# 132 matmuls on constant tiles ahead of the first real matmul of an attention and two-MLP kernel

## The chip, the cores and the metric

The kernel runs on one core of one Trainium2 chip. The metric is the device time of one execution in microseconds (us), the median of the runs made of it.

## The reference

Queries `q` of 12,288 tokens with 128 channels attend to 768 keys. The keys are the mean over 4 x 4 windows of `kv`, multiplied by `w_sr`, and serve as values too. The result goes through two MLPs of 128 -> 2048 -> 128, one with a ReLU whose negative side has a slope `alpha` per feature, one with a sigmoid approximation of GELU.

```python
kv_pool = kv.reshape(B, H // r, r, W // r, r, C).mean(axis=(2, 4))   # r = 4
k = v = kv_pool.reshape(B, -1, C) @ w_sr
a = softmax(q @ k.T / sqrt(C))
x = a @ v
h = x @ w_in;  y = (maximum(h, 0) + alpha * minimum(h, 0)) @ w_out
h = y @ w_in2; out = (h * sigmoid(1.702 * h)) @ w_out2
```

All tensors are float32.

## The kernel before, in words

Everything is held transposed, with the 128 channels on the partitions. The 12,288 tokens are worked off in 24 tiles of 512. Each of the five engines has one hand-written stream of instructions, and semaphores tie the streams together; nothing is reordered by a scheduler. So what stands first in an engine's stream holds up everything behind it on that engine.

A real product is made of three matmuls on float32r parts (`passes`, lines 639 to 641): high weights by high data, high by low, low by high. Each is 128 x 512 and brings a weight load of its own (engine PEld in the profile).

The program has a head and a loop. The head works in this order:

- SP loads `kvT` in 12 chunks of 512 KB into a ring of four buffers (`kv_raw`, line 234). From the fifth chunk on, each load waits until the chunk four before it has been reduced (`pooled_made`). Behind the last chunk come `w_in1`, `w_out1` and the second tile of queries (lines 241, 242, 245).
- DVE reduces each chunk to 64 keys (line 590). Behind chunk 3, 5, 7, 9 it makes the low parts of keys and values of a pair of chunks (`keys_values_lo`, lines 485 and 487), which waits for ACT's high parts. Behind chunk 4 it makes the high part of the first queries (line 480), from which POOL makes `q_lo` (line 277).
- PE multiplies each pair of chunks by `w_sr` (`keys_values`, lines 649 and 650, 128 x 128), and then makes the scores of the first query tile for the pair before (`scores`). ACT copies the products out and makes the high parts (lines 335, 336, 339).
- Then follow the maximum over the keys, the exponentials, attention of the first tile, the turned weights `w_in1` (line 772) and their product with `w_out1` (`mix`, line 701), and the first three `up` products, with which the steady part begins.

The loop then runs `tile` over the 24 tiles. In it the MLPs of tile t and the attention of tile t + 1 are interleaved on PE.

POOL begins its own stream with the identity matrix `ident` (memset at line 263, then 265), used by transposes much later. PE begins with `pe.wait_ge(small_in, 2 * DMA)` and `keys_values(0)`. The PSUM banks `ps_t` and `ps_y` (one bank each) are first used at lines 670 and 701.

Of the kernel before, what the change touches and what calls it, by code (L numbers as in the profile page):

```python
# [6 lines left out]
F32R = mybir.dt.float32r  # L7
# [4 lines left out]
P = 128  # L12
POOL = 4
WINDOW = POOL * POOL
TOK = 512
# [9 lines left out]
def attention_mlp_kernel(  # L25
# [53 lines left out]
    with ExitStack() as ctx:  # L79
        def sb(name, shape, dt=F32):  # L80
            return ctx.enter_context(nc.sbuf_tensor(name, shape, dt))

        def psum(name, shape):
            return ctx.enter_context(nc.psum_tensor(name, shape, F32))

        def sem(name):
            return ctx.enter_context(nc.semaphore(name))
# [4 lines left out]
        ps_t = psum("ps_t", [P, 512])  # L92
        ps_y = psum("ps_y", [P, 512])


        ident = sb("ident", [P, P])
        alpha_sb = sb("alpha_sb", [P, CH])
        one_less = sb("one_less", [P, CH])
# [53 lines left out]
        y_free = sem("y_free")  # L152
        mix_split = sem("mix_split")
        ident_made = sem("ident_made")
        warm_made = sem("warm_made")
        up1_hi_made = sem("up1_hi_made")
        pooled_made = sem("pooled_made")
# [46 lines left out]
        def f32(ap):  # L204
            return ap.bitcast(F32)
# [19 lines left out]
        @block.sync  # L225
        def _(sp):

            sp.sem_inc(out_free, DMA)
            for c in range(KV_CHUNKS):
                if c >= KV_RING:  # L230

                    sp.wait_ge(pooled_made, c - KV_RING + 1)
                src = kvT[:, c * KV_KEYS * WINDOW:(c + 1) * KV_KEYS * WINDOW]
                sp.dma_start(kv_raw[:, c % KV_RING].rearrange("p k w -> p (k w)"),
                             src).then_inc(kv_in[c % KV_RING], DMA)
                if c == 0:
                    sp.dma_start(wsr_sb[:], w_sr).then_inc(small_in, DMA)
                    sp.dma_start(alpha_sb[:], alpha).then_inc(small_in, DMA)
                if c == 1:
                    sp.dma_start(q_raw[:], qT[:, 0:TOK]).then_inc(q_in, DMA)  # L240
            sp.dma_start(w_raw[0][:], w_in1).then_inc(w_in[0], DMA)
            sp.dma_start(w_raw[1][:], w_out1).then_inc(w_in[1], DMA)

            sp.wait_ge(q_split, 1)
            sp.dma_start(q_raw[:], qT[:, TOK:2 * TOK]).then_inc(q_in, DMA)

            sp.wait_ge(w_hi, 1)
            sp.wait_ge(up0_lo_made, 1)
            sp.wait_ge(w_turned, RING)
            sp.dma_start(w_raw[0][:], w_in2).then_inc(w_in[2], DMA)  # L250

            sp.wait_ge(down0_lo_made, 1)
            sp.dma_start(w_raw[1][:], w_out2).then_inc(w_in[3], DMA)

            with sp.Fori(0, TILES - 2) as t:

                sp.wait_ge(q_split, t + 2)
                sp.dma_start(q_raw[:], qT[:, bass.ds(t * TOK + 2 * TOK, TOK)]).then_inc(q_in, DMA)


        @block.gpsimd
        def _(pool):
            nc.gpsimd.memset(ident[:], 0.0).then_inc(ident_made, 1)
            pool.wait_ge(ident_made, 1)
            nc.gpsimd.affine_select(out=ident[:], in_=ident[:], compare_op=ALU.not_equal, fill=1.0, base=0,
                                    pattern=[[-1, P]], channel_multiplier=1).then_inc(ident_made, 1)

            def scale_rows(src, factors, dst):

                src, dst = (w[:].rearrange("p (j c) -> p j c", j=CH) for w in (src, dst))  # L270
                by = factors[:].rearrange("p (j o) -> p j o", o=1).broadcast_to([P, CH, C])
                return nc.gpsimd.tensor_tensor(dst, src, by, ALU.mult)

            def queries_lo(u):

                pool.wait_ge(q_hi_made, u + 1)
                nc.gpsimd.tensor_tensor(q_lo[:], q_raw[:], f32(q_hi[:]), ALU.subtract).then_inc(q_split, 1)  # L277

            def subtract_max(u):

                pool.wait_ge(max_out, u + 1)
                for c in range(KC):
                    nc.gpsimd.tensor_tensor(s_sb[:, c, :], s_sb[:, c, :], max_sb[:], ALU.subtract).then_inc(  # L283
                        diff_done, 1)

            def sum_exponentials(u):
                for c in range(1, KC):

                    pool.wait_ge(exp_done, u * KC + (c + 1))
                    if c > 1:  # L290

                        pool.wait_ge(exp_sum_done, u * (KC - 1) + (c - 1))
                    nc.gpsimd.tensor_tensor(exp_sum[:], s_sb[:, 0, :] if c == 1 else exp_sum[:], s_sb[:, c, :],  # L293
                                            ALU.add).then_inc(exp_sum_done, 1)

            nc.gpsimd.memset(warm[:], 0.0).then_inc(warm_made, 1)
            queries_lo(0)

            pool.wait_ge(w_in[1], DMA)
            scale_rows(w_raw[1], alpha_sb, scaled).then_inc(w_scaled, 1)  # L300
            pool.wait_ge(alpha_made, 1)
            pool.wait_ge(w_scaled, 1)
            scale_rows(w_raw[1], one_less, w_raw[1]).then_inc(w_scaled, 1)

            sum_exponentials(0)
            queries_lo(1)

            pool.wait_ge(w_hi, 2)
            nc.gpsimd.tensor_tensor(down_lo[0][:], w_raw[1][:], f32(down_hi[0][:]), ALU.subtract).then_inc(
                down0_lo_made, 1)  # L310

            pool.wait_ge(up1_hi_made, 1)
            nc.gpsimd.tensor_tensor(up_lo[1][:], w_raw[0][:], f32(up_hi[1][:]), ALU.subtract).then_inc(mlp2_parts, 1)

            pool.wait_ge(w_in[3], DMA)
            nc.gpsimd.tensor_copy(down_hi[1][:], w_raw[1][:]).then_inc(mlp2_parts, 1)
            pool.wait_ge(mlp2_parts, 2)
            nc.gpsimd.tensor_tensor(down_lo[1][:], w_raw[1][:], f32(down_hi[1][:]), ALU.subtract).then_inc(
                mlp2_parts, 1)
            with pool.Fori(1, TILES - 1) as u:  # L320
                subtract_max(u)
                sum_exponentials(u)
                queries_lo(u + 1)
            subtract_max(TILES - 1)
            sum_exponentials(TILES - 1)
# [310 lines left out]
        def _(pe):  # L636
# [129 lines left out]
            def turn_w_in1(g):  # L766
# [5 lines left out]
                    step = nc.tensor.transpose(w_turn_bank(g)[:, cols(j % 4)], w_raw[0][:, cols(j)], ident[:])  # L772
                step.then_inc(w_turned, 1)

            pe.wait_ge(small_in, 2 * DMA)
            for c in range(KC):
                keys_values(c)
# [65 lines left out]
```

## Time and profile before

| what | us |
|---|---|
| median of the runs (2) | 1409.12 |
| lowest and highest | 1408.65, 1409.59 |
| span of the profiled execution, first to last instruction | 1407.1 |
| PE busy in it | 1365.1 (97%) |
| DVE busy | 1088.8 (77%) |
| ACT busy | 823.9 (59%) |
| POOL busy | 444.9 (32%) |

The profiled execution has 1407.1 us as its span; the median lies 2.0 us above it. A matmul's duration in the profile includes the part in which the next one already runs, so the time that a matmul costs in a stream is the distance between two starts. L with a number is the line of the kernel. PEclk is the granted clock of TensorE, 1.00 being 2.4 GHz and 0.50 being 1.2 GHz.

### The profile page before, as it was taken

What the parts mean: (1) busy time and instruction counts of PE and PEld (TensorE: products, weight loads), DVE (VectorE), ACT (ScalarE), POOL (GpSimd) and SP (SyncE); (2) the same over time, 40 slices, a digit from 0 to 9 for tenths busy, and PEclk for the clock granted to TensorE, in tenths of its full rate; (3) what the DMA queues carried; (4) which work ended last, traced back from release to release, by engine and by line L of the source; (5) the groups of instructions that cost most, each with busy time, mean ns of one, the idle gap of its engine ahead of it and who ended that gap; (6) DMA issues with size and microseconds to landing.
All of it is one profiled execution on the core that took longest, in us unless ns stands there. A gap on an engine that the chain in (4) does not pass through costs nothing.

```text
span 1407.1 us, 19487 instructions
## 1 busy us (share of the span) xinstructions
PE 1365.1 (97%) x6000; PEld 1094.6 (78%) x6000; DVE 1088.8 (77%) x1689; ACT 823.9 (59%) x1417; POOL 444.9 (32%) x295
## 2 busy tenths in 40 slices
PE   4599999999999999999999999999999999999998
PEld 3477887887887878878878788788787787887776
DVE  6868878778678787787786887877968877778775
ACT  2465665656656656656566566565665665655644
POOL 2740522413405314234054142241440522413400
PEclk8699999999999999999999999999999999999999
DMA  7100000000000000000000000000000000000000
GB/s 255 68 1 16 0 15 15 0 15 7 7 15 7 7 15 0 15 7 7 15 7 7 15 0 15 15 0 15 7 7 15 0 15 15 0 15 0 8 8 8
DMA packets 9514, 23.26 MB, mean 17 GB/s; under 512 B 1184, under 2 KB 1312, under 8 KB 8992
## 3 DMA queue, kind: packets, MB, share of 16 engines
q1 hardware_dynamic: 6048, 16.85, 3.6%
q10 hardware_dynamic: 3456, 6.29, 1.2%
q8 instruction: 4, 0.07, 0.0%
q14 instruction: 6, 0.05, 0.0%
HBM read 16.85 MB, written 6.29 MB: 16 GB/s over the span
## 4 chain that ended last, share of the span: by engine, by line
PE 90%; DVE 6%; ACT 1%; DMA 1%; issue 0%; SPq 0%; DVEq 0%; ACTq 0%
PE ps_y L639 14%; PE ps_y L641 13%; PE ps_y L640 13%; PE ps_h L641 12%; PE ps_h L639 12%; PE ps_h L640 12%; PE ps_s L639 4%; PE ps_s L640 4%; PE ps_s L641 4%; DVE g_lo L545 3%; PE ps_t L670 2%; PE ps_t L682 2%; DMA kv_raw<-kvT 1%; ACT g_full L372 1%; DVE g_hi L543 1%; DVE wide L502 0%
## 5 line engine op out<-in xcount | busy, mean ns | idle before, releaser
L283 POOL TENSOR_TENSOR s_sb<-s_sb,max_sb 128x512 f32<-128x512 f32 x138 | 205.3, 1523 | 577.6 <-ACT max_sb L349 577.6
L537 DVE SCALAR_TENSOR_TENSOR g_lo<-ps_h,g_hi 128x512 fp32r<-128x512 f32 x384 | 264.0, 688 | 153.1 <-ACT g_hi L367 150.5
L372 ACT ACTIVATE g_full<-ps_h 128x512 f32<-128x512 f32 x384 | 229.8, 598 | 252.6 <-PE ps_h L641 247.6
L545 DVE TENSOR_TENSOR g_lo<-g_full,g_hi 128x512 fp32r<-128x512 f32 x384 | 309.6, 806 | 13.1
L639 PE MATMUL ps_y<-g_hi,down_hi 128*128 128x512 f32 x768 | 313.4, 408 | 1.6 <-DVE g_lo L545 0.5
L641 PE MATMUL ps_y<-g_hi,down_lo 128*128 128x512 f32 x768 | 303.4, 395 | 0.0
L640 PE MATMUL ps_y<-g_lo,down_hi 128*128 128x512 f32 x768 | 302.4, 394 | 0.0
L367 ACT ACTIVATE g_hi<-ps_h 128x512 fp32r<-128x512 f32 x384 | 229.1, 597 | 94.2 <-PE ps_h L641 81.7
L543 DVE CAST g_hi<-g_full 128x512 fp32r<-128x512 f32 x384 | 161.9, 422 | 28.1 <-ACT g_full L372 28.0
L639 PEld LDWEIGHTS ps_y<-g_hi,down_hi 128*128 128x128 f32 x768 | 144.7, 188 | 47.7 <-DVE g_lo L545 18.6
L515 DVE TENSOR_TENSOR a_lo<-s_sb,a_hi 128x512 fp32r<-128x512 f32 x144 | 171.3, 1190 | 1.2 <-ACT a_hi L362 1.2
L641 PEld LDWEIGHTS ps_y<-g_hi,down_lo 128*128 128x128 f32 x768 | 144.3, 188 | 33.9
L640 PEld LDWEIGHTS ps_y<-g_lo,down_hi 128*128 128x128 f32 x768 | 144.7, 188 | 29.1
L639 PE MATMUL ps_h<-x_hi,up_hi 128*128 128x512 f32 x384 | 153.9, 401 | 1.6 <-DVE x_lo L551 1.6
L639 PE MATMUL ps_h<-y_hi,up_hi 128*128 128x512 f32 x384 | 151.1, 393 | 1.5 <-DVE y_lo L569 1.5
L641 PE MATMUL ps_h<-x_hi,up_lo 128*128 128x512 f32 x384 | 151.7, 395 | 0.0
L641 PE MATMUL ps_h<-y_hi,up_lo 128*128 128x512 f32 x384 | 151.6, 395 | 0.0
L640 PE MATMUL ps_h<-y_lo,up_hi 128*128 128x512 f32 x384 | 151.6, 395 | 0.0
L640 PE MATMUL ps_h<-x_lo,up_hi 128*128 128x512 f32 x384 | 151.0, 393 | 0.0
L293 POOL TENSOR_TENSOR exp_sum<-exp_sum,s_sb 128x512 f32<-128x512 f32 x96 | 142.0, 1479 | 10.7 <-ACT s_sb L354 2.6
L344 ACT COPY s_sb<-ps_s 128x512 f32<-128x512 f32 x144 | 84.5, 587 | 86.7 <-PE ps_s L641 74.7
L277 POOL TENSOR_TENSOR q_lo<-q_raw,q_hi 128x512 fp32r<-128x512 f32 x24 | 33.5, 1394 | 281.6 <-DVE q_hi L480 281.6
(90 smaller groups left out, 1774.9 us busy)
## 6 DMA issues: line engine op xcount, KB each, us to landing
kv_raw<-kvT SPq DMA_DIRECT2D x12, 512.0 KB, 5.4
q_raw<-qT SPq DMA_DIRECT2D x24, 256.0 KB, 2.6
outT<-out_sb ACTq DMA_DIRECT2D x24, 256.0 KB, 2.0
w_raw<-w_in SPq DMA_DIRECT2D x2, 1024.0 KB, 6.2
w_raw<-w_out SPq DMA_DIRECT2D x2, 1024.0 KB, 7.3
wsr_sb<-w_sr SPq DMA_DIRECT2D x1, 64.0 KB, 3.2
alpha_sb<-alpha SPq DMA_DIRECT2D x1, 8.0 KB, 3.5
```

The source lines that it names most:

```text
L283: nc.gpsimd.tensor_tensor(s_sb[:, c, :], s_sb[:, c, :], max_sb[:], ALU.subtract).then_inc(diff_done, 1)
L293: nc.gpsimd.tensor_tensor(exp_sum[:], s_sb[:, 0, :] if c == 1 else exp_sum[:], s_sb[:, c, :], ALU.add).then_inc(exp_sum_done, 1)
L344: nc.scalar.copy(s_sb[:, c, :], score_bank(c)).then_inc(scores_out, 1)
L367: nc.scalar.activation(g_hi[:, f % RING, :], ps_h[:, f % RING, :], ACT.Relu).then_inc(act_done, 1)
L372: nc.scalar.activation(g_full[:, f % RING, :], ps_h[:, f % RING, :], ACT.Gelu_apprx_sigmoid).then_inc(act_done, 1)
L515: nc.vector.tensor_tensor(a_lo[:, c % A_RING, :], s_sb[:, c, :], f32(a_hi[:, c % A_RING, :]), ALU.subtract).then_inc(a_split, 1)
L537: nc.vector.scalar_tensor_tensor(g_lo[:, f % RING, :], ps_h[:, f % RING, :], 0.0, f32(g_hi[:, f % RING, :]), ALU.max, ALU.subtract).then_i ...
L543: nc.vector.tensor_copy(g_hi[:, f % RING, :], g_full[:, f % RING, :]).then_inc(gelu_hi_made, 1)
L545: nc.vector.tensor_tensor(g_lo[:, f % RING, :], g_full[:, f % RING, :], f32(g_hi[:, f % RING, :]), ALU.subtract).then_inc(g_split, 1)
L639: nc.tensor.matmul(out, w_hi_ap, m_hi_ap, start=start, stop=False)
L640: nc.tensor.matmul(out, w_hi_ap, m_lo_ap, start=False, stop=False)
L641: return nc.tensor.matmul(out, w_lo_ap, m_hi_ap, start=False, stop=stop)
```

## The change

Two constant tiles are made by POOL ahead of the identity matrix: `probe_w`, two 128 x 128 weight tiles filled with 1.0, and `probe_m`, two 128 x 512 data tiles filled with 0.5. PE waits for both and then streams 132 matmuls of 128 x 512 on them into `ps_t` and `ps_y`, whose contents nothing reads. The six streams are:

1. 20 matmuls, weights in turn, one data tile, one bank;
2. 20 matmuls, weights and data in turn, one bank;
3. 20 matmuls, weights in turn, banks in turn;
4. 8 triples that accumulate like `passes`, banks in turn;
5. 8 triples with a semaphore signal behind each;
6. 8 triples with the signal and a wait that is already met.

Behind them the program of before goes on unchanged. No other engine's stream is changed.

```diff
+        probe_w = sb("probe_w", [P, 2, P], F32R)
+        probe_m = sb("probe_m", [P, 2, TOK], F32R)
         ident = sb("ident", [P, P])
...
+        probe_made = sem("probe_made")
+        probe_streamed = sem("probe_streamed")
...
         @block.gpsimd
         def _(pool):
+            nc.gpsimd.memset(f32(probe_w[:]), 1.0).then_inc(probe_made, 1)
+            nc.gpsimd.memset(f32(probe_m[:]), 0.5).then_inc(probe_made, 1)
             nc.gpsimd.memset(ident[:], 0.0).then_inc(ident_made, 1)
...
+            def stream(count, w, m, out):
+                for i in range(count):
+                    nc.tensor.matmul(out(i)[:], probe_w[:, w(i), :], probe_m[:, m(i), :], start=True, stop=True)
+
+            def triples(count, signal, wait):
+                for i in range(count):
+                    j = 0
+                    out = (ps_t, ps_y)[i % 2]
+                    if wait:
+                        pe.wait_ge(probe_made, 2)
+                    nc.tensor.matmul(out[:], probe_w[:, j, :], probe_m[:, j, :], start=True, stop=False)
+                    nc.tensor.matmul(out[:], probe_w[:, j, :], probe_m[:, j + 1, :], start=False, stop=False)
+                    step = nc.tensor.matmul(out[:], probe_w[:, j + 1, :], probe_m[:, j, :], start=False, stop=True)
+                    if signal:
+                        step.then_inc(probe_streamed, 1)
+
+            pe.wait_ge(probe_made, 2)
+            stream(20, lambda i: i % 2, lambda i: 0, lambda i: ps_t)
+            stream(20, lambda i: i % 2, lambda i: i % 2, lambda i: ps_t)
+            stream(20, lambda i: i % 2, lambda i: 0, lambda i: (ps_t, ps_y)[i % 2])
+            triples(8, False, False)
+            triples(8, True, False)
+            triples(8, True, True)
+
             pe.wait_ge(small_in, 2 * DMA)
             for c in range(KC):
                 keys_values(c)
```

The stream of PE at its very start, in the kernel before, with the semaphores that it waits for:

```order
L635 UNCONDITIONAL_BRANCH [waits barrier_Pool_Activation_PE_DVE_SP_release]
L649 MATMUL ps_h<-pooled,wsr_sb 128x128 [waits pooled_made,small_in]
L650 MATMUL ps_h<-wsr_sb,pooled 128x128
L649 MATMUL ps_h<-pooled,wsr_sb 128x128 [waits pooled_made]
L650 MATMUL ps_h<-wsr_sb,pooled 128x128
L639 MATMUL ps_s<-q_hi,k_hi 128x512 [waits kv_lo,q_split]
```

The same place in the changed kernel, whose lines 655, 656 and 645 are lines 649, 650 and 639 of before:

```order
L641 UNCONDITIONAL_BRANCH [waits barrier_Pool_Activation_PE_DVE_SP_release]
L784 MATMUL ps_t<-probe_m,probe_w 128x512 [waits probe_made]
L784 MATMUL ps_t<-probe_m,probe_w 128x512 x40
L784 MATMUL ps_y<-probe_m,probe_w 128x512
...
L792 MATMUL ps_y<-probe_m,probe_w 128x512 [waits probe_made]
L793 MATMUL ps_y<-probe_m,probe_w 128x512
L794 MATMUL ps_y<-probe_m,probe_w 128x512
L655 MATMUL ps_h<-pooled,wsr_sb 128x128 [waits pooled_made,small_in]
L656 MATMUL ps_h<-wsr_sb,pooled 128x128
L655 MATMUL ps_h<-pooled,wsr_sb 128x128 [waits pooled_made]
L656 MATMUL ps_h<-wsr_sb,pooled 128x128
L645 MATMUL ps_s<-q_hi,k_hi 128x512 [waits kv_lo,q_split]
```

The first `keys_values` product stands behind all 132 matmuls, in an unchanged order from there on.

The stream of DVE at its start, the same in both kernels, here in the kernel before; `kv_in` is a chunk's landing and `kv_hi` counts ACT's copies of PE's products:

```order
L472 UNCONDITIONAL_BRANCH [waits barrier_Pool_Activation_PE_DVE_SP_release]
L590 TENSOR_REDUCE pooled<-kv_raw 128x64 [waits kv_in0]
L600 TENSOR_SCALAR one_less<-alpha_sb 128x16 [waits small_in]
L590 TENSOR_REDUCE pooled<-kv_raw 128x64 [waits kv_in1]
L590 TENSOR_REDUCE pooled<-kv_raw 128x64 [waits kv_in2]
L590 TENSOR_REDUCE pooled<-kv_raw 128x64 [waits kv_in3]
L485 TENSOR_TENSOR k_lo<-k_full,k_hi 128x128 [waits kv_hi]
L487 SCALAR_TENSOR_TENSOR v_lo<-ps_h,v_hi 128x128
L590 TENSOR_REDUCE pooled<-kv_raw 128x64 [waits kv_in0]
L480 CAST q_hi<-q_raw 128x512 [waits q_in]
L590 TENSOR_REDUCE pooled<-kv_raw 128x64 [waits kv_in1]
```

Nothing moved here; the wait for `kv_hi` behind the fourth reduction is where DVE meets PE's first product.

## Rows read from the trace of the kernel before

**Rows 1.** The page: span, and busy time by engine.
```profile
span 1407.1 us, 19487 instructions
PE 1365.1 (97%) x6000; PEld 1094.6 (78%) x6000; DVE 1088.8 (77%) x1689; ACT 823.9 (59%) x1417; POOL 444.9 (32%) x295
```

**Rows 2.** Busy time by stretch: PE, PEld, DVE, ACT, POOL (count), PEclk, DMA, GB/s.
```profile
60.00:75.00 15.00, 9.18 (x43) 8.37 (x44) 11.47 (x7) 3.16 (x6) 10.27 (x3) 0.77 0.25 88
75.00:100.00 25.00, 25.00 (x113) 20.35 (x112) 18.19 (x26) 16.69 (x31) 10.67 (x8) 1.00 0.00 1
```

**Rows 3.** Chain that ended last, 0 to 60 us: start, duration, what.
```profile
3.62 7.25 DMA kv_raw<-kvT
...
24.71 1.22 DVE pooled L590
```

**Rows 4.** Timeline of 0 to 20 us: start, duration, engine, line, operation.
```profile
0.74 0.20 POOL L263 MEMSET ident<- 128x128 f32 x1 [0.29 <-POOLq L836]
...
1.43 0.10 POOL L296 MEMSET warm<- 128x1 f32 x1
...
8.64 0.76 PE L649 MATMUL ps_h<-pooled,wsr_sb 128*128 128x128 f32 x2 [8.64 <-DVE pooled L590]
...
9.62 2.49 DVE L590 TENSOR_REDUCE pooled<-kv_raw 128x64 f32<-128x1024 f32 x2 [1.13 <-DMA kv_raw<-kvT]
9.92 1.28 ACT L335 ACT_TABLE_LOAD   x1 [9.92 <-PE ps_h L650]
...
12.23 0.28 DVE L487 SCALAR_TENSOR_TENSOR v_lo<-ps_h,v_hi 128x128 fp32r<-128x128 f32 x1
12.43 1.21 DVE L590 TENSOR_REDUCE pooled<-kv_raw 128x64 f32<-128x1024 f32 x1
...
14.06 1.26 POOL L277 TENSOR_TENSOR q_lo<-q_raw,q_hi 128x512 fp32r<-128x512 f32 x1 [12.54 <-DVE q_hi L480]
15.02 0.45 DVE L485 TENSOR_TENSOR k_lo<-k_full,k_hi 128x128 fp32r<-128x128 f32 x1
15.38 0.29 PEld L639 LDWEIGHTS ps_s<-q_hi,k_hi 128*128 128x128 f32 x1 [2.28 <-POOL q_lo L277]
...
16.82 0.63 PE L649 MATMUL ps_h<-pooled,wsr_sb 128*128 128x128 f32 x2
...
18.25 0.30 ACT L339 CAST k_hi<-k_full 128x128 fp32r<-128x128 f32 x1
...
19.61 0.43 SPq L241 DMA_DIRECT2D w_raw<-w_in  x1
```

**Rows 5.** PE's timeline in the loop, first and last of 37 matmuls.
```profile
599.63 0.39 PE L640 MATMUL ps_y<-g_lo,down_hi 128*128 128x512 f32 x1
...
607.99 0.39 PE L640 MATMUL ps_s<-a_lo,v_hi 128*128 128x512 f32 x1
```

**Rows 6.** PE's timeline in the head at the low clock.
```profile
49.02 0.63 PE L640 MATMUL ps_s<-a_lo,v_hi 128*128 128x512 f32 x1
...
49.45 0.63 PE L641 MATMUL ps_s<-a_hi,v_lo 128*128 128x512 f32 x1
```

**Rows 7.** Timeline of the head: where bursts of PE begin, and line 641 at 21.14.
```profile
21.14 0.46 PE L641 MATMUL ps_s<-q_hi,k_lo 128*128 128x512 f32 x1
...
46.13 0.80 PE L639 MATMUL ps_s<-a_hi,v_hi 128*128 128x512 f32 x1 [1.28 <-DVE a_lo L515]
...
64.20 1.12 PE L682 MATMUL ps_t<-ident,wide 128*128 128x128 f32 x4 [7.28 <-DVE wide L502]
```

**Rows 8.** Busy time by stretch of 1 us (columns as in rows 2), two queries.
```profile
55.00:56.00 1.00, 1.00 (x6) 0.81 (x6) 0.74 (x2) 0.00 (x0) 1.00 (x1) 0.80 0.00 0
...
69.00:70.00 1.00, 0.84 (x7) 0.65 (x6) 1.00 (x1) 0.13 (x1) 1.00 (x1) 0.97 0.00 0
```

**Rows 9.** DMA issues on the page: count, size, median us to landing.
```profile
kv_raw<-kvT SPq DMA_DIRECT2D x12, 512.0 KB, 5.4
```

**Rows 10.** Costliest groups on the page: a weight load of the second MLP product.
```profile
L641 PEld LDWEIGHTS ps_y<-g_hi,down_lo 128*128 128x128 f32 x768 | 144.3, 188 | 33.9
```

## The prediction, made before the changed kernel ran

> **What bounds the kernel now.** I read the page first. The span is 1407.1 us and PE is busy in 97% of it [rows 1]. Next the busy time by stretch: from 75 us on PE is busy without a gap (25.00 of 25.00 us) at granted clock 1.00, while between 60 and 75 us it has work for 9.18 of 15 us [rows 2]. So there are two regimes. In the loop PE is the bound, and whatever arrives late at the loop's door moves the end by as much. In the head PE mostly waits, and delay on it may be swallowed. The change stands in the head, so the question is how much slack the head has ahead of PE's first product. The chain that ended last says what the head hangs on: the landing of the kv chunks from 3.62 us (a piece of 7.25 us first), up to the twelfth reduction, DVE's at 24.71 us, ending at 25.93 [rows 3]. Last I read the timeline of the first 20 us to see which engine feeds which [rows 4].
>
> **The change part by part.** Nothing is removed. Added are two memsets on POOL, 132 matmuls with their weight loads on PE, and a wait of PE for the memsets.
>
> *Memsets.* POOL's memset of 128 columns takes 0.20 us, that of 1 column 0.10, so about 0.10 fixed and 0.8 ns a column [rows 4]. 256 columns give 0.30 and 1024 give 0.91 us. They begin where `ident` began, at 0.74, so PE starts its stream near 0.74 + 0.30 + 0.91 + 0.05 = 2.0 us. POOL's subtraction over 512 columns takes 1.26 us, 2.5 ns a column [rows 4]; at that rate the memsets end at 3.9, the upper bound; the lower is 1.0, were they done as fast as `ident`'s. I take 2.0, since the same operation is the nearest row. `ident` and all else on POOL come about 1.2 us later, hidden: POOL idles from 1.5 to 14.06, waiting for DVE [rows 4].
>
> *A matmul at the high clock.* In the loop 37 starts in a row lie between 599.63 and 607.99: 8.36 / 36 = 0.232 us each [rows 5]. They are the same 128x512 with one weight load each, so I take 0.232. Below, 512 columns at 2.4 GHz are 0.213 us. Above, if each had to end before the next starts, it would be the row's duration of 0.39; the rows speak against that, since starts lie closer than durations.
>
> *A matmul at the low clock.* Starts at 49.02 and 49.45, so 0.43 [rows 6]; 512 columns at 1.2 GHz are 0.427.
>
> *How long the stream runs at the low clock.* A burst that begins at 64.20 after 7.28 us of idleness runs unbroken, and in the stretch 69 to 70 the granted clock is 0.97, which puts the rise at 69.06: 4.9 us [rows 7, 8]. A burst with gaps beginning at 46.13 saw the rise in 55 to 56 (0.80: at 55.4), 9.3 us on. The first rise must come near 21.1, where line 641 shortens from 0.63 to 0.46 us [rows 7], 5.8 us behind the scores' start at 15.38. What stands recorded as 1.00 before that can't be so: spacings there are those of 1.2 GHz. I take 4.9 us, the unbroken burst being nearest to a stream without gaps; bounds 0 and 9.3.
>
> *The six streams together.* 4.9 us hold 11.4 matmuls at 0.427. The other 120.6 at 0.232 take 28.0 us. Together 32.9 us; PE is free at T = 2.0 + 32.9 = 34.9 us. Order of weights, data and banks, the signals and the met waits I cost at nothing: real triples with different operands, banks, signals and waits already run at 0.232.
>
> The Trainium skill, "TensorE: Matmul & The Clock Gate", section "Wait — 56ns, not 53.3ns?", says that back-to-back starts at the full clock lie N / 2.4 GHz plus about 2.5 ns apart, 215.7 ns at N = 512. The loop's 0.232 doesn't agree. By the page's figure the stream would be about 2.0 us shorter; that is the first rival below.
>
> *What the delay of the first product costs.* PE's first product moves from 8.64 to 34.9 [rows 4], 26.3 us. Part comes back, since four chunks are already reduced, and four more landed, when PE arrives. DVE ends its fourth reduction at 9.62 + 2.49 = 12.1 as before, and then stands at `keys_values_lo(0)`, which needs ACT, which needs PE. Behind DVE the eight other reductions wait, behind those SP's loads of chunks 8 to 11, and behind these both weight loads. I replay the head with durations of before [rows 4], counted from T:
>
> - first product at the high clock done at 0.65 (low: 9.92 - 8.64 = 1.28). ACT's table load and copies, then `v_lo` ends at 12.51 - 9.92 = 2.6 later, less 0.2 since DVE isn't late: 3.1.
> - reduction 5, `q_hi`, reduction 6 as before (12.51 to 15.02): 5.6. `q_lo` starts 1.55 after `v_lo`'s end and takes 1.26: scores begin at 6.0.
> - `keys_values_lo(1)` 0.45, reductions 7 and 8: 8.5. `keys_values_lo(2)` needs the third pair's `k_hi`, 18.55 - 15.38 = 3.2 after the scores' start, at the low clock: 9.2.
> - to 9.65; two reductions to 12.1; `keys_values_lo(3)` to 12.55; the last two reductions to 15.0.
>
> Do the loads keep up? The loads of chunks 8 to 11 are issued at 4.3, 5.6, 7.3 and 8.5. At the median of 5.4 us to landing, which they had under full traffic [rows 9], they land at 9.7, 11.0, 12.7 and 13.9, against use at 9.65, 10.9, 12.55 and 13.8: at most 0.2 us late. The load of `w_in1` follows 6.1 us ahead of the last reduction's end; before it was 25.93 - 19.61 = 6.3 [rows 3, 4]. So from there on the head is as it was.
>
> The last reduction ends at 34.9 + 15.0 = 49.9 instead of 25.93: +24.0 us, and 2.3 of the 26.3 us come back. The rest of the head, the loop and the end are the same, all later by 24.0. Phases of the clock in the head may add or take 1.5 us.
>
> **The sum.** 1407.1 + 24.0 = 1431.1 us of span, and with the 2.0 us by which the median stands above this span, 1433.1 us, 1.7% over 1409.1. A change of 2%, about what a measurement of this kernel can tell from no change, is 28.2 us: 1437.3.
>
> **The rivals.**
>
> *The stream runs at 0.213.* The loop's extra 0.019 us would then come from signals, waits or traffic of other engines, which plain constants lack. Against it: nothing in the timeline sits between the 37 starts, and triples are among the probes. 120.6 x 0.019 is 2.3 us less: 1430.8 us. Chance 0.15.
>
> *The starts come closer than 512 columns at 2.4 GHz.* If two matmuls could overlap until the weight load bounds them, its 0.188 us [rows 10], the 120.6 take 22.7 instead of 28.0 us and the time is 1427.8. Against it: the loop's dense rows keep 0.232 with the same weight load. Chance 0.02. The Trainium skill, the same page, section "Back-to-back issue gap", gives 131 ns a matmul at N = 512 as sustained; an estimate by that page would be 1421 us. The loop's 0.232 [rows 5] disagrees with it.
>
> *The clock stays low, on the slower side.* Were the clock not raised in the stream, or taken back within it, each matmul costs 0.427: all 132 take 56.4 us, T is 58.4 and the time 1433.1 + 23.5 = 1456.6. It passes 1437.3 as soon as the low clock lasts 9 us longer than my 4.9, about 14 us in all. For it: the clock fell in the head several times and a rise came after 9.3 us once. Against it: the stream has no gap, and in the loop the clock stays at 1.00. Chance 0.07.
>
> *The head swallows less.* If the shift of 26.3 us comes through whole, 1435.4 us. If late memsets (+1.9 us), a late rise (+2.0) and late chunks come on top, it goes to 1439. Chance 0.15.
>
> *The head swallows all.* It would need the chain of landings to stay the later of the two. But T lies 9 us behind the last reduction of before, and eight reductions and all scores still come behind T. 1409 us. Chance 0.01.
>
> **How the numbers follow.** The forecast with its own spread (1432 to 1435) has 0.60. The range goes from the fast stream with an early rise, 1428.5, to late memsets and a late rise together, 1439. It leaves out the low clock, the closest starts and the swallowed delay, and a small rest of the others. Slower by over 2%: 0.07 for the low clock, 0.05 of the case of the head that swallows less, 0.01 of the rest, 0.13. Faster by over 2%: nothing is taken off the path, 0.01. Within 2%: 0.86.
>
> **What would show it.** Right: PE's first probe near 2 us; starts of 0.43 for some 5 us, then 0.232 in all six streams; the first product of line 655 near 35 us; four reductions by 12 us, then DVE idle until about T + 2.6; the last reduction near 50; the loop's spacing unchanged and every stage later by the same 24 us. Wrong: a stream that differs from the others in spacing, a granted clock of 0.50 past 14 us, a late last chunk, or a loop whose length changes. A shift at the loop's door other than 24 us while T is 35 would refute the replay of the head.

## The result, and the profile after

The changed kernel takes 1431.91 us (median of 2 runs, 1431.54 to 1432.29) against 1409.12: ratio 1.0162, 95% interval 1.0143 to 1.0181. It is 22.8 us slower, where 24.0 were forecast, inside the range of 1428.5 to 1439. The profiled execution spans 1430.5 us (forecast 1431.1) instead of 1407.1.

The page of the changed kernel, span and busy time, against [rows 1]:

```profile
span 1430.5 us, 19753 instructions
PE 1394.5 (97%) x6132; PEld 1119.2 (78%) x6132; DVE 1087.6 (76%) x1689; ACT 824.2 (58%) x1417; POOL 445.8 (31%) x297
```

PE has 132 instructions more. Its share is 97% as before, which shows why a share says nothing about usefulness: the added matmuls count as busy. DVE and ACT have the same work as before and POOL two memsets more; their busy times moved by at most 1.2 us.

Its timeline at the very start, against [rows 4]:

```profile
0.74 0.31 POOL L267 MEMSET probe_w<- 128x256 f32 x1 [0.29 <-POOLq L867]
...
0.99 0.96 POOL L268 MEMSET probe_m<- 128x1024 f32 x1
...
2.00 10.21 PE L784 MATMUL ps_t<-probe_m,probe_w 128*128 128x512 f32 x36 [2.00 <-POOL probe_m L268]
```

The memsets took 0.31 and 0.96 us (0.30 and 0.91 forecast), and PE starts at 2.00 as forecast.

The stream, in PE's timeline: two starts at its beginning, the first start of the triples and the last, and the first real product, which is line 649 of before:

```profile
2.59 1.05 PE L784 MATMUL ps_t<-probe_m,probe_w 128*128 128x512 f32 x2
...
3.02 1.05 PE L784 MATMUL ps_t<-probe_m,probe_w 128*128 128x512 f32 x2
...
17.49 0.39 PE L792 MATMUL ps_t<-probe_m,probe_w 128*128 128x512 f32 x1
...
33.58 0.40 PE L794 MATMUL ps_y<-probe_m,probe_w 128*128 128x512 f32 x1
33.81 0.39 PE L655 MATMUL ps_h<-pooled,wsr_sb 128*128 128x128 f32 x2
```

At first starts lie 0.43 us apart. The 72 matmuls of the triples begin between 17.49 and 33.58: 16.09 / 71 = 0.2266 us, in all three kinds. The second and third stream, between 8.42 and 12.73 and between 12.95 and 17.26, have the same 4.31 / 19 = 0.227. In the order of weights, data and banks, in signals and in met waits there is no difference to be seen, at a resolution of one nanosecond. But 0.227 is less than the loop's 0.232 [rows 5].

How long the low clock lasted is told by the starts one by one; the number of matmuls under way in a stretch shows it too (PE busy and count, PEclk, DMA share, GB/s):

```profile
5.00:6.00 1.00, 1.00 (x4) 1.00 1.01 340
6.00:7.00 1.00, 1.00 (x6) 1.00 1.01 313
```

The spacing changes at 5.8 us, after 3.8 us of stream, not 4.9. PEclk says 1.00 from the start, which the starts refute, just as in the kernel before: it holds nothing ahead of the first recorded change. PE is free at T = 33.8 instead of 34.9.

Now the replay of the head. This is the chain that ended last, from the first product on (start, duration, what):

```profile
34.51 1.28 ACT L341
...
36.96 1.13 DVE pooled L596
38.09 0.33 DVE q_hi L486
38.42 1.13 DVE pooled L596
39.55 0.37 DVE k_lo L491
...
40.12 2.26 DVE pooled L596 x2
...
42.40 6.46 DMA kv_raw<-kvT
...
48.88 1.22 DVE pooled L596
```

Up to 42.4 it is the replay nearly to the tenth: `v_lo` done at T + 3.15 (3.1 forecast), the scores' start at T + 6.0 (6.0). Then a landing stands in the chain, on which DVE waited:

```profile
48.88 1.22 DVE L596 TENSOR_REDUCE pooled<-kv_raw 128x64 f32<-128x1024 f32 x1 [1.43 <-DMA kv_raw<-kvT]
```

DVE waited 1.43 us for the last chunk, and the last reduction ends at 50.1, T + 16.3 where 15.0 were forecast. T was 1.1 us early and the replay 1.3 us late, so the last reduction came within 0.2 us of the forecast 49.9. The first `up` product, with which the loop's work begins, starts at 95.39, before at 71.45: 23.9 us later, 24.0 forecast. From there to the end the profiled execution of the changed kernel is some 0.6 us quicker; what makes up that difference wasn't looked for.

### The profile page after: what moved, and what is told of

The parts are those of the page before. It is cut to its first block, busy times and chain, and to the rows that moved or that the text cites. A ratio compares the mean times of both kernels' runs of the same rounds, so it can differ in the third digit from the quotient of the medians.

```text
span 1430.5 us, 19753 instructions
## 1 busy us (share of the span) xinstructions
PE 1394.5 (97%) x6132; PEld 1119.2 (78%) x6132; DVE 1087.6 (76%) x1689; ACT 824.2 (58%) x1417; POOL 445.8 (31%) x297
## 4 chain that ended last, share of the span: by engine, by line
PE 92%; DVE 5%; ACT 1%; DMA 0%; issue 0%; POOL 0%; ACTq 0%; DVEq 0%; POOLq 0%
PE ps_y L645 13%; PE ps_y L647 13%; PE ps_y L646 13%; PE ps_h L647 12%; PE ps_h L645 12%; PE ps_h L646 12%; PE ps_s L645 4%; PE ps_s L646 4%; PE ps_s L647 4%; DVE g_lo L551 2%; PE ps_t L676 2%; PE ps_t L688 1%; PE ps_t L784 1%; ACT g_full L378 1%; DVE g_hi L549 1%; DMA kv_raw<-kvT 0%
```

## The experiments

**How the price depends on the length of the stream.** Four kernels, timed in three rounds beside the kernel before (1409.26 us).

```diff
             pe.wait_ge(probe_made, 2)
-            stream(20, lambda i: i % 2, lambda i: 0, lambda i: ps_t)
-            stream(20, lambda i: i % 2, lambda i: i % 2, lambda i: ps_t)
-            stream(20, lambda i: i % 2, lambda i: 0, lambda i: (ps_t, ps_y)[i % 2])
-            triples(8, False, False)
-            triples(8, True, False)
-            triples(8, True, True)
```

This is `memsets_only`, without any stream. `n20` keeps the first line, `n60` the first three, and `n264` has all six lines twice.

`memsets_only` was expected so:

> The change without its 132 matmuls: the two memsets on POOL and PE's wait for them stay. Theory (all of the time is the stream on PE, and POOL idles to 14 us): 1409.1 us within 1, PE's first product at 8.6 us as before. Rival (some of the 22.8 us come from the memsets, the shifted tiles or the longer program): over 1411 us.

`n20`:

> Only the first stream, 20 matmuls; in the changed kernel the 20th starts near 8.2 us, so PE is free at about 8.4, ahead of the second reduction. Theory (the head swallows a stream that ends before its first product could start): 1409.1 us within 1, last reduction ends near 26 us. Rival (each matmul costs its own 0.227 us wherever it stands): 8.4 - 2.0 = 6.4 us more, 1415.5.

`n60`:

> Three streams, 60 matmuls: PE free at 17.5 us in the changed kernel's trace. Theory (behind the end of the stream, T, the head needs 16.3 us to the last reduction's end, as in the changed kernel, where T is 33.8 and the end 50.1): last reduction ends at 33.8, 7.9 us later than before, 1417 us. With the 15.0 us of my replay it would be 32.5 and 1415.7. Rival (whole shift of the first product, 17.5 - 8.6): 1418.0.

`n264`:

> All six streams twice, 264 matmuls. Theory (every further matmul costs 0.2267 us at the high clock, nothing of it hidden): 132 x 0.2267 = 29.9 us above the changed kernel, 1461.8 us, and the clock stays at 1.00 from 6 us to the end of the stream. Rival (the clock is taken back in a long stream of constants, or part is swallowed): above 1465 or below 1458.

| kernel | us | ratio, 95% interval | first product | last reduction ends |
|---|---|---|---|---|
| memsets_only | 1408.92 | 0.9998 (0.9988 to 1.0007) | 9.2 | 25.4 |
| n20 | 1409.34 | 1.0001 (0.9991 to 1.001) | 10.0 | 27.0 |
| n60 | 1416.35 | 1.0052 (1.0035 to 1.0069) | 17.6 | 33.8 |
| changed, 132 | 1431.91 | 1.0162 (1.0143 to 1.0181) | 33.8 | 50.1 |
| n264 | 1463.05 | 1.0381 (1.0364 to 1.0399) | 64.4 | 80.8 |

The first products of `memsets_only` and `n20` start later than the 8.6 us of before because the second chunk landed later in these executions. The memsets and the moved tiles cost nothing. Twenty matmuls, 6.8 us of PE, cost nothing either. In the trace of `n20` the stream is over and PE still waits for DVE's second reduction, which itself waited for its chunk:

```profile
7.70 1.30 PE L784 MATMUL ps_t<-probe_m,probe_w 128*128 128x512 f32 x5
...
8.67 1.22 DVE L596 TENSOR_REDUCE pooled<-kv_raw 128x64 f32<-128x1024 f32 x1 [2.79 <-DMA kv_raw<-kvT]
...
10.03 0.46 PE L655 MATMUL ps_h<-pooled,wsr_sb 128*128 128x128 f32 x2 [1.03 <-DVE pooled L596]
```

With 60 the last reduction ends 16.3 us behind T, with 132 too, with 264 at 16.4. So the price of the stream is nothing as long as T + 16.3 stays under 26, that is T under about 9.7 us. That is an estimate from the traces; `n20`, whose stream ends at 8.8, lies below it, and no run lies between 8.8 and 17.5. Beyond it each microsecond of T costs a whole one. T less the price in the median time is 10.5, 11.0 and 10.6 us in the three longer kernels, so by the times the free part reaches nearly a microsecond further.

Of the rivals in the expectation of `n60`, the whole shift (1418.0) lies above all its runs (1415.95 to 1416.57). The theory's 1417 lies just above them and the replay's 15.0 (1415.7) just below, so the time doesn't decide between these two; the last reduction's end in the trace does, with 33.8 as the theory said and not 32.5.

`n264` came 1.3 us above its 1461.8. In its profiled execution the clock rose later:

```profile
6.00:7.00 1.00, 1.00 (x4) 0.80 (x3) 0.03 (x1) 0.00 (x0) 0.00 (x0) 1.00 0.93 231
7.00:8.00 1.00, 1.00 (x6) 0.82 (x5) 0.10 (x1) 0.00 (x0) 0.00 (x0) 1.00 0.82 277
```

Four matmuls under way between 6 and 7 us against six in the changed kernel: the low clock lasted to 7.2. By the price below that is 0.7 us of the 1.3; the rest has no cause shown. Over the six profiled executions that have such a stream at the start it ended between 5.8 and 7.9 us, 3.8 to 5.9 us into the stream. A microsecond of it costs 1 - 0.227 / 0.427 = 0.47 us. Up to the rise PE's stream is the same in all six, so what a kernel adds behind it can't be the reason; no kernel was profiled twice, so that it is scatter between executions is the likely reading and not a measured one.

**Why the replay took 16.3 and not 15.0.** Eight kv buffers instead of four, four of them in `g_full` and `scaled`, which are unused at that time, so that the last loads no longer wait for reductions that stand behind PE; timed beside the kernel before (1409.60), without the stream too.

```diff
-KV_RING = 4
+KV_RING = 8
...
+            pool.wait_ge(pooled_made, 8)
             pool.wait_ge(w_in[1], DMA)
             scale_rows(w_raw[1], alpha_sb, scaled).then_inc(w_scaled, 1)
```

> The changed kernel with eight kv buffers instead of four, four of them in tiles that are free at that time. Theory (behind the stream the last chunk's late landing, on which DVE waits 1.43 us, is what made the head's replay 16.3 instead of 15.0 us): the last reduction starts 1.4 us earlier, ends near 48.7, 14.9 us behind T, and the time falls by about 1.4 us to 1430.5. Rival (something else than the landing makes up the difference): last reduction still near 50.1, 1431.9.

> The kernel before with eight kv buffers, no stream. Theory (the head before hangs on landings of kv chunks that were issued late or share the engines with the weights): all 12 chunks are issued in a row ahead of the weights, DVE becomes the bound, the last reduction ends at 22 to 23.5 instead of 25.9 and the time falls by 2 to 4 us, to 1405 to 1407. Rival (the 16 engines carry no more anyway, or the weights that land later take the gain back): 1409.

Both theories fell. `ring_after` took 1432.80 us (1.0164, 1.0148 to 1.0179), `ring_before` 1409.26 (1.0001, 0.9992 to 1.001): its last reduction ended at 24.8, 1.1 us sooner, but its first `up` started at 72.1, not sooner than before. There POOL's scaling began at 26.84, and beside it a later `k_lo` took 3.69 us and two running maxima 4.82, which gave the gain back. The landings did come early in `ring_after`, no reduction behind T waited for one; but its last reduction ended at 53.4, 18.6 us behind its T of 34.8. DVE's and POOL's timeline there:

```profile
43.44 3.61 POOL L286 TENSOR_TENSOR scaled<-w_raw,alpha_sb 128x2048 f32<-128x2048 f32 x1 [2.68 <-DVE pooled L605]
```
```profile
44.01 3.19 DVE L500 TENSOR_TENSOR k_lo<-k_full,k_hi 128x128 fp32r<-128x128 f32 x1 [0.65 <-ACT k_hi L354]
```

`w_out1` had long landed, so the eighth reduction, for which the new wait stands, let POOL begin its long scaling in the middle of the kv work. DVE's `k_lo` of 0.29 us took 3.19 and ended at 47.20, just after POOL's piece at 47.05. So I held POOL back.

```diff
-            pool.wait_ge(pooled_made, 8)
+            pool.wait_ge(chunk_max_done, KC - 1)
```

> The changed kernel with eight kv buffers, as in ring_after, and POOL's scaling of w_out held back until the last running maximum, so that it can't stand beside DVE's work on keys. Theory (in ring_after DVE's low parts took 3.19 and 1.38 us instead of 0.3 because POOL scaled beside them; without that the replay is bound by DVE alone): k_lo at 0.3 us, last reduction ends 14.9 to 15.2 us behind the stream's end instead of 18.6, last running maximum not stretched; time 1428 to 1430.5. Rival (DVE's long pieces have another cause): they stay.

`ring_hold`: the last reduction ends at 49.0 with T at 34.4, so 14.6 us behind T. Without late landings and without POOL, DVE's own work is the bound of the replay, as forecast. Yet the time is 1433.83 (1.0173, 1.0158 to 1.0189): nothing is gained.

```profile
55.17 3.61 POOL L286 TENSOR_TENSOR scaled<-w_raw,alpha_sb 128x2048 f32<-128x2048 f32 x1 [14.78 <-DVE running_max L510]
58.92 3.61 POOL L286 TENSOR_TENSOR w_raw<-w_raw,one_less 128x2048 f32<-128x2048 f32 x1
```
```profile
58.98 5.70 DVE L627 TENSOR_TENSOR up_lo<-w_raw,up_hi 128x2048 fp32r<-128x2048 f32 x1
```

POOL's two pieces now stand beside `up_lo`, which takes 5.70 us; in the kernel before it took 2.28. The stretch moved to the next piece of DVE. The first `up` starts at 96.1, 0.7 us later than in the changed kernel; 0.6 us of that is the later T, so the 1.7 us that the replay gained are gone again.

These rows also say what the stretch is. `up_lo` ends at 64.68, which is 2.15 us behind the end of POOL's first piece (62.53), nearly its own 2.28. `k_lo` above ends 0.15 us behind POOL's piece, with 0.29 of its own; `denom` of the kernel before, which begins at 55.95 beside a piece of POOL that ends at 59.41, ends 0.03 us behind it, with 0.17 of its own. So the DVE piece isn't slowed: it stands until POOL's piece is over and then needs its own time less some 0.14 us. What it costs is the rest of POOL's piece. Not every DVE instruction is held: in `ring_after` two reductions took 2.33 us from 47.32 on, as they do elsewhere, while POOL's second piece ran from 47.19 to 50.80.

**A version that beats both.** If an early stream is free until the head needs PE, such matmuls may go into PE's gaps and keep the clock up. Timed in five rounds beside the kernel before (1409.60).

```diff
+            pe.wait_ge(fill_made, 2)
+            fill(18, ps_t[:])
             pe.wait_ge(small_in, 2 * DMA)
...
             scores(0, KC - 1)
+            fill(12, ps_t[:])
             pe.wait_ge(ident_made, 2)
             turn_max(0)
...
                 attend(0, c)
+                if c < KC - 2:
+                    fill(5, ps_y[:])
...
             mix(range(CH // 4))
+            fill(27, ps_h[:, 0, :])
             spread(inv_wide, 0, inv_spread)
```

(and 8, 9, 8, 9 and 13 more in other gaps: 124 in all)

> The kernel before with the same kind of constant matmuls, about 130 of them, laid into PE's idle gaps of the head in pieces of 0.9 to 6.4 us, each sized to end before PE's next input. Theory (a stream costs nothing where PE has nothing else to do, and keeps the granted clock at 1.00, which shortens PE's pieces of the chain at 29.0, 34.2, 37.9, 52.7 and 64.2 us by 3.5 us in all): 1405.5 us, granted clock 1.00 nearly all along the head. Rival (fillers run into the inputs and delay them, or the clock isn't held by them): 1409 or above.

1404.80 us, ratio 0.9969 (0.9959 to 0.9979): nearly as many matmuls as in the change, and the kernel is quicker than before by 4.8 us. Busy time by stretch, PE to POOL, PEclk, DMA, GB/s:

```profile
30.00:45.00 15.00, 11.12 (x59) 8.53 (x58) 13.26 (x10) 6.50 (x10) 9.71 (x4) 1.00 0.20 71
45.00:60.00 15.00, 14.47 (x67) 10.95 (x66) 13.06 (x12) 9.12 (x12) 11.27 (x6) 1.00 0.00 0
```

The granted clock is 1.00; in the kernel before it was 0.61 and 0.66 in the same stretches. The first `up` starts at 67.34, 4.1 us sooner. The expected 1405.5 was nearly met, but not by the 3.5 us that it took from PE's own pieces. Only part is PE's own; the rest is an engine that slips ahead of another. DVE's timeline:

```profile
53.66 0.69 DVE L526 TENSOR_REDUCE col_sum<-ps_t 128x4 f32<-128x512 f32 x1 [0.56 <-PE ps_t L675]
54.39 0.17 DVE L528 TENSOR_SCALAR denom<-col_sum 128x4 f32<-128x4 f32 x1
```

The sums come at 53.66 instead of 55.23, ahead of POOL's long piece that begins at 54.43, and `denom` takes 0.17 us; before it stood beside that piece and took 3.49. Next `wide` takes 4.52 beside POOL all the same, but it ends at 59.33 instead of 64.15: DVE waits out one long piece of POOL there and not two. A second such piece is `x_lo`, which released the first `up` in the kernel before. It stood beside POOL's second `down_lo`; with the gaps filled it is done before that begins. Before, and in `fill_gaps`:

```profile
66.80 4.50 DVE L551 TENSOR_TENSOR x_lo<-x_full,x_hi 128x512 fp32r<-128x512 f32 x1 [0.68 <-ACT x_hi L383]
```
```profile
63.30 1.01 DVE L556 TENSOR_TENSOR x_lo<-x_full,x_hi 128x512 fp32r<-128x512 f32 x1 [0.69 <-ACT x_hi L388]
```

So the sums come 1.6 us sooner, `wide` is done 4.8 us sooner and `x_lo` 7.0 us sooner. Of this the first `up` gets only 4.1, because the last fillers run into it. PE's timeline:

```profile
64.26 3.25 PE L782 MATMUL ps_h<-fill_m,fill_w 128*128 128x512 f32 x13
67.34 0.40 PE L644 MATMUL ps_h<-x_hi,up_hi 128*128 128x512 f32 x1
```

`x_lo` was done at 64.31. Without these 13 fillers up to some 2.9 us more might be gained, an estimate from these rows that no run tests. How much of the 4.8 us is the clock's by itself and how much the order of DVE and POOL isn't separated by a run either.

To take the remaining stretch from the running maximum I held POOL back here too:

> The filled gaps of fill_gaps, and POOL's scaling held back until the last running maximum. Theory (beside POOL's scaling the last running maximum took over 2 us instead of 0.7): 2 us less than fill_gaps, 1402.8. Rival (the stretch moves to DVE's next pieces, or POOL is late for the sums): 1404.8 or above.

1410.09 us (1.0004, 0.9995 to 1.0013), 5.3 us worse than `fill_gaps` and against the theory. The last running maximum does fall from 3.28 to 0.69 us. But `up_lo` rises to 5.70, the sums arrive at 57.19, `denom` takes 3.56 again and `x_lo` 5.00. And while DVE stood, PE had nothing to do:

```profile
45.84 0.77 PE L645 MATMUL ps_s<-a_hi,v_hi 128*128 128x512 f32 x1 [4.90 <-DVE a_lo L521]
```

Behind these 4.90 us the granted clock is 0.50 between 45 and 50 us, where `fill_gaps` has 1.00, and the fillers between the attention products, now at 0.43 us each, delay what stands behind them. Holding POOL back is no gain in either kernel.

**Why 0.227 in the streams and 0.232 in the loop.** Three kernels, one execution each.

```diff
             scores(0, KC - 1)
...
+            plain(30, 512)
+            real(30)
+            plain(31, 256)
+            for phase in range(5):
+                nc.tensor.matmul(ps_t[:], probe_w[:, 0, :], probe_m[:, 0, :], start=True,
+                                 stop=True).then_inc(probe_streamed, 1)
+                plain(34, 512)
```

The definitions, the loops of the other engines and the removal of the six streams are left out here. `plain` runs on constants, `real` with `k_hi`, `k_lo` as weights and `q_hi`, `q_lo` as data. The signal of each phase sets one engine to work: ACT copying from PSUM, DVE copying from PSUM, DVE adding in SBUF, POOL adding in SBUF, none.

> The six streams are taken out; behind the scores of the head stand 30 matmuls on constants, 30 on real keys and queries (eight weight tiles in turn), 31 constants of 256 columns, and five runs of 35 constants: beside ACT copying PSUM banks, DVE copying PSUM, DVE adding in SBUF, POOL adding in SBUF, and alone. Only starts of matmuls are read. In the changed kernel all six streams start every 226.7 ns, in the loop 230 to 233. Theory A (other engines' traffic costs the extra 5 ns): 226.7 alone, 230 or more beside one of the engines. Theory B (real operands cost it): 226.7 everywhere but 230 or more on keys and queries. Theory C (neither; it is the loop's own waits and instructions between matmuls): 226.7 in all. If a weight load adds a fixed time of 13.3 ns to 512 / 2.4, 256 columns start every 120 ns.

PE's timeline, first and last of the real ones, and 256 columns:

```profile
39.63 0.39 PE L829 MATMUL ps_t<-q_hi,k_hi 128*128 128x512 f32 x1
...
46.21 0.40 PE L829 MATMUL ps_y<-q_lo,k_lo 128*128 128x512 f32 x1
46.44 0.28 PE L834 MATMUL ps_t<-probe_m,probe_w 128*128 128x256 f32 x1
...
50.04 0.28 PE L834 MATMUL ps_t<-probe_m,probe_w 128*128 128x256 f32 x1
```

Real operands: 6.58 / 29 = 0.227. Beside DVE in PSUM, DVE in SBUF, POOL and alone: 0.2267 each; beside ACT 0.2275, with only the first five starts wider (228 to 236 ns), while ACT copied for 6 us. These five aren't ACT's doing: the first two, 233 and 236 ns, begin before ACT's first copy at 50.59, and 236, 228, 233 and 230 ns also stand behind the rise of the clock in the changed kernel, where ACT is idle. So no one engine's traffic and no real data alone make the 0.232. The 31 matmuls of 256 columns start 3.60 / 30 = 0.120 apart. From 256 to 512 columns it is 0.1067 us more, which is 256 / 2.4 GHz, and 13.3 ns are left at either size: a fixed price of each of these matmuls, each of which has its own weight load. No run here goes without the weight loads, so whether the price is theirs isn't shown.

```diff
+                    if lag and i >= lag:
+                        pe.wait_ge(echo, base + i - lag + 1)
```

> Four runs of 20 triples on constants in the head. In the first no wait; in the others PE waits before triple i for DVE's answer to triple i - 2, i - 3, i - 6. Theory (the loop's 232 ns come from waits that are met only shortly before the matmul, so that PE's instructions can't run ahead): 226.7 without waits, 230 to 236 at a distance of 2 or 3, 226.7 again at 6. Rival (something else in the loop): 226.7 in all four, apart from stalls at a distance of 2.

226.7 ns in all, at distances 2, 3 and 6. At distance 2 DVE's answer was there only 0.31 us ahead of the matmul that waits for it, at 3 0.99 us: waits met late, but met, cost nothing. The theory fell.

```diff
-                passes(ps_h[:, f % RING, :], up_hi[m][:, cols(f)], up_lo[m][:, cols(f)], src_hi[:], src_lo[:],
+                passes(ps_h[:, f % RING, :], probe_w[:, 0, :], probe_w[:, 1, :], probe_m[:, 0, :], probe_m[:, 1, :],
```

(and the same for `down`)

> The six streams are taken out, and in the loop all up and down products (4608 of the matmuls) take their weights and data from the constant tiles, so that the MLPs aren't computed; every wait, signal and instruction of the other engines stays, and scores and attention keep their operands. Theory A (the loop's 231 to 233 ns against 226.7 in the streams come from the operands, which change and are freshly written): up and down start every 227 ns, scores and attention every 231, and the time falls by up to 4608 x 5 ns = 23 us, to 1386. Theory B (they come from the loop itself, its waits, other engines' traffic all at once): 231 to 233 for all, 1409.

1399.59 us against 1408.17, one run each, over a third of what theory A allowed. Leaving out the stalls above 260 ns, the up and down products start every 228 to 229 ns on average, most often 226 or 227; before it was 231 to 234, on average 232.4. The stalls between 150 and 1350 us grew at the same time, from 17.4 to 24.0 us, which is why less of it is seen in the total. Scores and attention, whose operands stayed, remain at 227 to 236. Neither theory holds whole: about two thirds of the extra go when up and down get constants, the rest doesn't.

Nor is it the matmul's own operands alone. These are the first of nine constant `up` products between attention products in `loop_const`, and the attention product behind them:

```profile
602.82 0.40 PE L645 MATMUL ps_h<-probe_m,probe_w 128*128 128x512 f32 x1
...
604.91 0.39 PE L645 MATMUL ps_s<-a_hi,v_hi 128*128 128x512 f32 x1
```

They take 2.09 / 9 = 0.232, on constants. And in the loop of before, the wider starts come round in a cycle, over attention, down and up products alike:

```profile
600.32 0.40 PE L640 MATMUL ps_s<-a_lo,v_hi 128*128 128x512 f32 x1
600.56 0.40 PE L641 MATMUL ps_s<-a_hi,v_lo 128*128 128x512 f32 x1
...
601.94 0.40 PE L641 MATMUL ps_y<-g_hi,down_lo 128*128 128x512 f32 x1
602.18 0.40 PE L639 MATMUL ps_y<-g_hi,down_hi 128*128 128x512 f32 x1
```

Between 600 and 608 us every seventh distance is 241 ns, the six others 228 to 233. So 0.227 and 0.232 look like two rhythms of PE, of which the unbroken streams here soon reach the quicker one. What brings PE into one or the other stays open.

## Why the prediction was right

- *Memsets and start*: 2.0 forecast, 2.00 measured; `memsets_only` shows that they are hidden.
- *Low clock*: 4.9 taken, 3.8 in this execution, 0.5 us too much. Six executions gave 3.8 to 5.9, so 4.9 was a fair middle.
- *Spacing at the high clock*: 0.232 taken from the loop, 0.2267 measured. Over 121 matmuls that is 0.6 us too much. The rival of 0.213 fell as well, since it lacked the fixed 13.3 ns. By the Trainium skill ("TensorE: Matmul & The Clock Gate", "Wait — 56ns, not 53.3ns?") that fixed part is about 2.5 ns, 215.7 ns in all; these float32r matmuls with a weight load each don't agree, with 226.7.
- *T*: 34.9 forecast, 33.8 measured, the sum of the two terms above.
- *Replay of the head*: 15.0 forecast, 16.3 measured. The step that failed was "do the loads keep up?". I gave each of the last four loads the median of 5.4 us; they took 3.8, 4.3, 4.9 and 6.5, so it was the last alone that came too late. All four and the weights behind them were issued within 5.6 us, which is the likely reason, though no run tests it. `ring_hold`, where that wait is gone, needs 14.6.
- *The rest shifts by the same amount*: 23.9 us at the first `up`, 24.0 forecast.
- *The rivals*: the clock stayed up in 132 and in 264 matmuls; the head did swallow 1.2 us of the first product's shift of 25.2 (2.3 of 26.3 were forecast); closer starts weren't seen.

The two errors had opposite signs, 1.1 and 1.3 us, so the total is better than its terms, and that is luck. Of the 23.9 us, 0.6 are lost again between the first `up` and the end, the rest of the way to 22.8 is the difference between a median and a profiled execution.

## What to carry to other kernels

Work added to an engine in front of its first input is free up to the moment when that input would be used, and costs its full length beyond; find that moment in the timeline, then replay the head from there with the queues behind each wait (here DVE, then SP's loads). Nearly the same matmuls that cost 22.8 us in one block gained 4.8 us when cut to the gaps: they held the clock, and DVE's pieces came to stand ahead of POOL's long ones. Moving a long POOL piece away from one DVE piece only helps if the next DVE piece isn't held instead, and if PE doesn't idle long enough behind it to lose the clock.

## What was not expected of the hardware

- A 128x512 float32r matmul with its own weight load starts every 226.7 ns at 2.4 GHz and a 128x256 one every 120.0: columns / 2.4 GHz + 13.3 ns, by these two sizes. At the low clock the spacing is 427 ns, with no such addition.
- In the loop it is 231 to 233 ns. With constants for up and down part of the addition goes (1399.6 us against 1408.2, one run each), yet constants right behind attention products keep 0.232.
- The time to the rise of the clock in an unbroken stream varied from 3.8 to 5.9 us between executions, worth about 1 us of total time.
- A DVE instruction that begins beside a long POOL instruction may stand until that one ends and then take its own time: `k_lo` 3.19 instead of 0.29 us, `denom` 3.49 instead of 0.17, `up_lo` 5.70 instead of 2.28. Reductions of `kv_raw` beside POOL kept their duration.
